# Queries with no matching key: scale and bias zero in the exponential, in place of a mean of v made by GpSimd and TensorE

## What is computed

```
q_bits = (q @ proj > 0);  k_bits = (k @ proj > 0)
mask = q_bucket[:, :, :, None] == k_bucket[:, :, None, :]
scores = where(mask, q @ k.T / sqrt(D), -1e9)
scores = scores - max(scores, axis=-1)
attn = exp(scores)
attn = attn / (sum(attn, axis=-1) + 1e-9)
out = attn @ v
```

## Time and profile before

| | |
|---|---|
| median of 3 runs | 767.33 us (766.6 to 768.45) |
| profiled execution, time | 768.82 us |
| its span, first to last instruction | 767.0 us |
| busy: TensorE, VectorE, ScalarE, GpSimd | 656.2, 425.9, 341.4, 340.7 us |
| attention in the span | 0 to 276 us |
| mean granted TensorE clock | 0.924 of full |

### The profile page before, as it was taken

The page is one execution under the profiler, slowest core; times in us unless marked ns, Lnnn a source line. Parts: engine busy times, 40 slices in busy tenths (PEclk is TensorE's granted clock), DMA queues, the critical chain, the costliest instruction groups (busy, mean ns, idle before and its releaser), DMA issues. The chain is left out here.

```text
span 767.0 us, 10365 instructions
## 1 busy us (share of the span) xinstructions
PE 656.2 (86%) x3758; PEld 521.2 (68%) x3759; DVE 425.9 (56%) x568; ACT 341.4 (45%) x528; POOL 340.7 (44%) x204
## 2 busy tenths in 40 slices
PE   2999999999999879108799999999576899889998
PEld 0666666666666569108699998898455688668886
DVE  6877787877875321604265545661169884632222
ACT  2766666766656623005055533451245463612200
POOL 4573753936632046253266444660156545723300
PEclk9999999999999975557899999999878999989999
DMA  9105162360632045145565667711352202122311
GB/s 302 42 1 171 42 214 73 142 208 6 212 132 109 1 184 199 71 178 170 189 228 201 210 213 244 246 44 41 109 194 71 68 0 83 41 83 83 109 42 56
DMA packets 50975, 96.09 MB, mean 125 GB/s; under 512 B 16624, under 2 KB 16624, under 8 KB 50928
## 3 DMA queue, kind: packets, MB, share of 16 engines
q1 hardware_dynamic: 48720, 88.38, 33.7%
q0 software_dynamic: 1920, 6.29, 2.3%
q10 hardware_dynamic: 288, 0.79, 0.3%
HBM read 69.23 MB, written 26.21 MB: 124 GB/s over the span
## 5 line engine op out<-in xcount | busy, mean ns | idle before, releaser
L879 POOL TENSOR_TENSOR w_lo<-stage,w_hi 128x1024 fp32r<-128x1024 f32 x28 | 85.1, 3058 | 92.0 <-ACT w_hi L874 92.0
L250 ACT COPY probs_t<-turned 128x768 f32<-128x768 f32 x96 | 76.8, 800 | 68.4 <-PE turned L427 63.5
L312 DVE TENSOR_REDUCE neg_max<-scores 128x1 f32<-128x768 f32 x96 | 91.6, 955 | 26.4 <-PE scores L418 24.5
L258 ACT ACTIVATE probs<-scores,neg_max 128x768 f32<-128x768 f32 x96 | 86.9, 905 | 23.4 <-DVE neg_max L312 23.3
L427 PE MATMUL turned<-ident,probs 128*128 128x128 f32 x576 | 80.7, 276 | 13.7 <-ACT probs_t L250 13.6
L427 PEld LDWEIGHTS turned<-ident,probs 128*128 128x128 f32 x576 | 65.6, 142 | 29.8 <-issue 28.2
L968 PE MATMUL up<-xt_hi,w_hi 128*128 128x256 f32 x256 | 75.7, 296 | 7.7 <-issue 5.7
L968 PE MATMUL up<-xt_hi,w_lo 128*128 128x256 f32 x256 | 75.0, 293 | 0.0
L968 PE MATMUL up<-xt_lo,w_hi 128*128 128x256 f32 x256 | 75.0, 293 | 0.0
L439 PE MATMUL pv<-probs_t,v_in 128*64 128x384 f32 x384 | 72.3, 498 | 0.8 <-DVE out_t L319 0.8
L418 PE MATMUL scores<-k_aug,q_aug 76*128 76x384 f32 x192 | 59.7, 393 | 9.5 <-DVE k_aug L305 8.7
(11 more groups left out here) (170 smaller groups left out, 1420.8 us busy)
## 6 DMA issues: line engine op xcount, KB each, us to landing
stage<-in_w SPq DMA_DIRECT2D x64, 512.0 KB, 4.6
wt_raw<-in_w_tok SPq DMA_DIRECT2D x12, 768.0 KB, 4.5
x_slots<-zeros SPq DMA_DIRECT2D x7, 1024.0 KB, 8.6
y_slots<-zeros SPq DMA_DIRECT2D x7, 1024.0 KB, 10.4
q_raw<-in_qT SPq DMA_DIRECT2D x16, 384.0 KB, 5.2
k_raw<-in_kT SPq DMA_DIRECT2D x14, 384.0 KB, 5.8
x_in<-x_slots SPq DMA_DIRECT2D x10, 512.0 KB, 5.1
y_slots<-y_out SPq DMA_DIRECT2D x8, 512.0 KB, 2.8
```

The source lines that it names most:

```text
L250: nc.scalar.copy(probs_t[j % 2][:, a, :, t % 3 * P:(t % 3 + 1) * P].rearrange("k (b n) q -> k b n q", b=2), turned[:, :, 0:HALF].rearrange ...
L258: nc.scalar.activation(probs[g % 3][:].rearrange("p (b n) -> p b n", b=2), scores[g % 2][:, :, 0:HALF], ACT.Exp, bias=neg_max[:, pair, a, ...
L312: nc.vector.tensor_reduce(neg_max[:, pair, a, t:t + 1], scores[g % 2][:, :, 0:HALF], AX.XY, ALU.max, negate=True).then_inc(s_max, 1)
L879: name.tensor_tensor(w_lo[w][:, r, :], stage[:, r, :], w_hi[w][:, r, :].bitcast(F32), ALU.subtract).then_inc(done, 1)
```

## The change

`exponential` gets a scale for each query beside the bias. After each `maximum` VectorE makes two values for each query: `match` (1 where the maximum is above `FLOOR`, else 0) and `bias` (`neg_max` times the same). For a query without a match the exponential is then exp(0 * score + 0) = 1 for every key, its sum 768, and the ordinary path gives the mean of v. `maximum` signals a new semaphore, `s_neg`, for which VectorE itself waits before the two small instructions; `s_max` counts those two. Everything that made and added the mean goes: `sum_v`, `add_fallback`, the matmul with `ones`, `v_mean`, `no_match`, the multiplication in `reciprocals`, and their buffers, semaphores and waits.

```diff
@@ -58,18 +58,14 @@
     q_hl = of_heads("q_hl", [P, S], F32R)
     k_lh = of_heads("k_lh", [P, S], F32R)
     v_in = [sb(f"v_in{p}", [P, 2, T, D]) for p in range(2)]
-    v_add = sb("v_add", [P, 2, 3, D])
-    v_sum = sb("v_sum", [P, 2, D])
-    v_mean = sb("v_mean", [P, 2, D])
-    fallback = sb("fallback", [P, T, 2, D])
     probs = [sb(f"probs{n}", [P, S]) for n in range(3)]
     probs_t = [sb(f"probs_t{n}", [P, 2, T, HALF]) for n in range(2)]
     out_t = [sb(f"out_t{n}", [P, HALF]) for n in range(2)]
     neg_max = sb("neg_max", [P, NPAIRS, 2, T])
     total = sb("total", [P, NPAIRS, 2, T])
-    no_match = sb("no_match", [P, 2, T])
+    match = sb("match", [P, NPAIRS, 2, T])
+    bias = sb("bias", [P, NPAIRS, 2, T])
     recip = sb("recip", [P, 2, T])
-    ones = sb("ones", [P, P])
     proj_raw = sb("proj_raw", [P, NBITS])
     w_bits = sb("w_bits", [P, 2 * NBITS])
     thresh = [sb("thresh_q", [P, 1]), sb("thresh_k", [P, 1])]
@@ -140,7 +133,7 @@
         for pair in range(2):
             load_v(pair)
         load_routing(sp)
-        sp.wait_ge(s_constp, 4)
+        sp.wait_ge(s_constp, 3)
         for n in range(2):
             clear(sp, None, n)
         for pair in range(NPAIRS):
@@ -158,7 +151,6 @@
                     clear(sp, pair - 1, n)
             if pair + 2 < NPAIRS:
                 sp.wait_ge(s_pv, 2 * pair + 2)
-                sp.wait_ge(s_vadd, 3 * pair + 1)
                 load_v(pair + 2)
 
     @block.gpsimd
@@ -167,7 +159,6 @@
         pool.wait_ge(s_constp, 1)
         nc.gpsimd.affine_select(out=ident[:], in_=ident[:], compare_op=ALU.not_equal, fill=1.0, base=0,
                                 pattern=[[-1, P]], channel_multiplier=1).then_inc(s_constp, 1)
-        nc.gpsimd.memset(ones[:], 1.0).then_inc(s_constp, 1)
         nc.gpsimd.memset(zeros[:], 0.0).then_inc(s_constp, 1)
 
         def q_high(pair, a):
@@ -191,30 +182,6 @@
                 pool.wait_ge(s_khi, 2 * pair + a + 1)
             nc.gpsimd.tensor_tensor(k_lh[p][a][0:D, :], k_raw[p][a][0:D, :], k_aug[p][a][0:D, :].bitcast(F32),
                                     ALU.subtract).then_inc(s_klo, 1)
-
-        def sum_v(pair):
-            p = pair % 2
-            pool.wait_ge(s_klo, min(2 * pair + 4, NHEADS))
-            pool.wait_ge(s_v[p], 32 * (pair // 2) + 32)
-            nc.gpsimd.tensor_tensor(v_add[:], v_in[p][:, :, 0:3, :], v_in[p][:, :, 3:6, :], ALU.add).then_inc(s_vadd, 1)
-            pool.wait_ge(s_vadd, 3 * pair + 1)
-            nc.gpsimd.tensor_tensor(v_add[:, :, 0, :], v_add[:, :, 0, :], v_add[:, :, 1, :], ALU.add).then_inc(s_vadd, 1)
-            pool.wait_ge(s_vadd, 3 * pair + 2)
-            if pair > 0:
-                pool.wait_ge(s_vmean, pair)
-            nc.gpsimd.tensor_tensor(v_sum[:], v_add[:, :, 0, :], v_add[:, :, 2, :], ALU.add).then_inc(s_vadd, 1)
-
-        def add_fallback(pair):
-            pool.wait_ge(s_vmean, pair + 1)
-            pool.wait_ge(s_rec, 4 * pair + 4)
-            if pair > 0:
-                pool.wait_ge(s_x, pair)
-            nc.gpsimd.tensor_tensor(fallback[:], v_mean[:].unsqueeze(1).to_broadcast([P, T, 2, D]),
-                                    no_match[:].rearrange("q a t -> q t a").unsqueeze(3).to_broadcast([P, T, 2, D]),
-                                    ALU.mult).then_inc(s_fall, 1)
-            pool.wait_ge(s_fall, pair + 1)
-            pool.wait_ge(s_norm, 2 * pair + 2)
-            nc.gpsimd.tensor_tensor(x_of(pair), x_of(pair), fallback[:], ALU.add).then_inc(s_x, 1)
 
         k_low(0, 1)
         pool.wait_ge(s_qhi, 2)
@@ -227,10 +194,6 @@
                     q_high(pair + 1, a)
                     k_high(pair + 1, a)
                     k_low(pair + 1, a)
-            sum_v(pair)
-            if pair > 0:
-                add_fallback(pair - 1)
-        add_fallback(NPAIRS - 1)
 
     @block.scalar
     def _(act):
@@ -252,11 +215,11 @@
 
         def exponential(g):
             pair, a, t = place(g)
-            act.wait_ge(s_max, g + 1)
+            act.wait_ge(s_max, 2 * g + 2)
             if g >= 3:
                 act.wait_ge(s_tp, g - 2)
             nc.scalar.activation(probs[g % 3][:].rearrange("p (b n) -> p b n", b=2), scores[g % 2][:, :, 0:HALF], ACT.Exp,
-                                 bias=neg_max[:, pair, a, t:t + 1],
+                                 bias=bias[:, pair, a, t:t + 1], scale=match[:, pair, a, t:t + 1],
                                  accum_out=total[:, pair, a, t:t + 1]).then_inc(s_exp, 1)
 
         for g in range(STEPS + TURN_LAG):
@@ -310,7 +273,13 @@
             pair, a, t = place(g)
             dve.wait_ge(s_sc, g + 1)
             nc.vector.tensor_reduce(neg_max[:, pair, a, t:t + 1], scores[g % 2][:, :, 0:HALF], AX.XY, ALU.max,
-                                    negate=True).then_inc(s_max, 1)
+                                    negate=True).then_inc(s_neg, 1)
+
+            dve.wait_ge(s_neg, g + 1)
+            nc.vector.tensor_scalar(match[:, pair, a, t:t + 1], neg_max[:, pair, a, t:t + 1], -FLOOR, None,
+                                    ALU.is_le).then_inc(s_max, 1)
+            nc.vector.scalar_tensor_tensor(bias[:, pair, a, t:t + 1], neg_max[:, pair, a, t:t + 1], -FLOOR,
+                                           neg_max[:, pair, a, t:t + 1], ALU.is_le, ALU.mult).then_inc(s_max, 1)
 
         def evict_out(j):
             dve.wait_ge(s_pv, j + 1)
@@ -322,23 +291,14 @@
             dve.wait_ge(s_exp, 12 * pair + 12)
             if pair > 0:
                 dve.wait_ge(s_norm, 2 * pair)
-                dve.wait_ge(s_fall, pair)
             nc.vector.tensor_scalar_add(recip[:], total[:, pair, :, :], 1e-9).then_inc(s_rec, 1)
-            nc.vector.tensor_scalar(no_match[:], neg_max[:, pair, :, :], -FLOOR, 1.0 / S, ALU.is_gt, ALU.mult).then_inc(s_rec, 1)
-            dve.wait_ge(s_rec, 4 * pair + 1)
+            dve.wait_ge(s_rec, 2 * pair + 1)
             nc.vector.reciprocal(recip[:], recip[:]).then_inc(s_rec, 1)
-            dve.wait_ge(s_rec, 4 * pair + 3)
-            nc.vector.scalar_tensor_tensor(recip[:], neg_max[:, pair, :, :], -FLOOR, recip[:], ALU.is_le,
-                                           ALU.mult).then_inc(s_rec, 1)
 
         def normalise(j):
             pair, half = divmod(j, 2)
             dve.wait_ge(s_ot, j + 1)
-            dve.wait_ge(s_rec, 4 * pair + 4)
-            if half == 0:
-                if pair > 0:
-                    dve.wait_ge(s_fall, pair)
-                nc.vector.tensor_copy(v_mean[:].rearrange("q a d -> q (a d)"), side[:, HALF:512]).then_inc(s_vmean, 1)
+            dve.wait_ge(s_rec, 2 * pair + 2)
             tiles = slice(3 * half, 3 * half + 3)
             nc.vector.tensor_tensor(x_of(pair, tiles), side[:, 0:HALF].rearrange("q (t a d) -> q t a d", t=3, a=2),
                                     recip[:, :, tiles].rearrange("q a t -> q t a").unsqueeze(3).to_broadcast([P, 3, 2, D]),
@@ -399,7 +359,6 @@
             j = max(0, (g - TURN_LAG + 5) // 6)
             if j > 0:
                 pe.wait_ge(s_norm, j)
-                pe.wait_ge(s_vmean, (j + 1) // 2)
 
         def score(g):
             pair, a, t = place(g)
@@ -443,15 +402,12 @@
 
         def turn_out(j):
             pe.wait_ge(s_oev, j + 1)
-            if j % 2 == 0:
-                pe.wait_ge(s_vadd, 3 * (j // 2) + 3)
-                nc.tensor.matmul(side[:, HALF:512], ones[:], v_sum[:].rearrange("p a d -> p (a d)"), start=True, stop=True)
             for n in range(3):
                 last = nc.tensor.transpose(side[:, n * P:(n + 1) * P], out_t[j % 2][:, n * P:(n + 1) * P], ident[:])
             last.then_inc(s_ot, 1)
 
         pe.wait_ge(s_const, N_CONSTS)
-        pe.wait_ge(s_constp, 3)
+        pe.wait_ge(s_constp, 2)
         for a in range(2):
             pe.wait_ge(s_qk[0][a], 32)
             for of_k in range(2):
```

More of the change, by code:

```diff
@@ L96, in attention @@
     s_sc = sem("s_sc")
+    s_neg = sem("s_neg")
     s_max = sem("s_max")
@@ L105, in attention @@
     s_norm = sem("s_norm")
[L106 to L109, removed]
     block = ctx.enter_context(nc.Block())
```

## The result

The changed kernel takes 756.25 us (median of 4 runs, 755.32 to 756.76); the kernel before took 767.84 us beside it. The ratio is 0.9848, 95% interval 0.9832 to 0.9864: 11.6 us faster, where 2.1 us were forecast and the range ended at 762.8. The profiled execution took 756.28 us.

A forecast was written before the change was run, and what follows sets the result against it. TensorE was taken to pace attention, with later stages untouched. The terms -2.2 - 1.95 + 0.9 + 1.1 were summed to -2.1 us, giving 765.3 us on the median of 767.33; the range was 762.8 to 771.5.

The forecast's parts named there:

- Mean's matmuls: TensorE in attention: turning out without the mean's matmul saves 0.27 us for each of 8 pairs, 2.2 us.
- Last addition: End of attention: GpSimd's last addition of the mean, all on the path, goes and saves 1.95 us.
- Start: Start of attention: TensorE waits for each exponential, so delays from the small instructions aren't hidden; 1.1 us lost, between 0.4 and 2.1.
- Ends of pairs: Step 11 of a pair: small instructions held behind GpSimd's L177 delay the waiting score, 0.15 us at six places, 0.9 us.
- first rival: VectorE's one-element instructions are not held while GpSimd works; all but 0.4 us is covered, 763.6 us; chance 0.18.
- The reading that both kinds are held: VectorE in attention: both kinds of small instruction, seen held with 12 elements, wait until GpSimd's instruction is over.
- second rival: GpSimd's next instruction starts before VectorE's second small one, which waits up to 2.3 us more; 769.7 to 774 us; chance 0.25.
- the third: Rival: the two small instructions cost VectorE 0.5 us, not 0.27, in each step; +3.3 us, 768.6 us; chance 0.15.
- Second operand of the exponential: ScalarE in attention: a scale from memory beside the bias adds between 0 and 0.11 us to each exponential, taken as 0.1.

The follow-up runs named there:

- cheaper bias: The changed kernel with the bias made by tensor_scalar with two scalars in place of scalar_tensor_tensor, same values; 756.37 us (ratio 0.9856).
- changed + 47: The changed kernel with 94 satisfied waits (47 instructions) behind routing's last matmul, in TensorE's idle time; 764.48 us (ratio 0.9959).
- first try: The changed kernel with 47 satisfied waits (24 instructions by the page) at the head of the experts' TensorE program; 760.92 us (ratio 0.9903).
- with the matmul: The changed kernel with one unread TensorE matmul of the mean's shape before every second turning-out, 16 instructions more; 763.89 us (ratio 0.9936).

## Why the prediction was wrong

The step that failed is this one: "The stages after attention start when its last engine is done and are not touched: what attention gains or loses is what the program does." Attention gained 3.5 us and the experts 8.4, and the latter through the number of instructions that stand ahead of them in TensorE's program. That is shown both ways: 47 idle instructions make the changed kernel's stage 8.8 us longer, 209 make that of the kernel before 9.5 us shorter. The forecast costed every instruction that goes by its duration and none by its place. What would have made the forecast wrong was named ("so does a later stage that changes its own length"), without a rival or a chance for it, although the row with 3.97 us of idle time for "issue" stood in the trace of before.

The sum itself is -2.15 us and so 765.2 us, written as -2.1 and 765.3. Its terms, by the table above:

- **Mean's matmuls, -2.2: right.** First to last eviction fell by 2.26 us; the matmul alone brings 2.20 back. Where the earlier trace rows had 0.57 us to the next score there are now 0.31.
- **Last addition, -1.95: right,** 1.98. The kernel before without that addition alone has 2.40 us from the last eviction to the end, 1.72 less; the other 0.25 goes with the rest of GpSimd's last wait. The next stage follows 0.33 us after the last normalisation (0.34 forecast):

```profile
273.02 0.56 DVE L303 TENSOR_TENSOR x_all<-side,recip 128x384 f32<-128x384 f32 x1 [0.70 <-PE side L406]
...
273.91 1.07 PE L704 MATMUL banks<-ident,x_all 128*128 128x128 f32 x8 [0.93 <-PEq L1365]
```

- **Start, +1.1: 0.6 to 0.9.** The first exponential starts at 20.87 in place of 20.27, the second at 22.00 in place of 21.55. The first eviction comes 0.8 us later than in the kernel before and 0.9 later than without the small instructions, but it moves by up to 0.9 us between traces of one kernel, roughly with the moment at which the granted clock rises to 1.00; where that moment is 26.6 to 26.8 us, the difference is 0.6 to 0.7 (50.25 before, 50.80 and 50.94 changed).
- **Ends of pairs, +0.9: nothing.** A pair takes 31.05 us, 0.29 less than in the earlier trace rows and just the mean's share (31.07 was given for the case that all is covered); without the small instructions first to last is the same 220.5.

```profile
113.33:144.38 31.05, 29.76 (x191) 19.48 (x192) 26.55 (x55) 21.79 (x37) 11.73 (x9) 1.00 0.41 132
```

The term took the small instructions of step 11 to be held behind L177, L168 in the changed kernel. There they are not held, and the exponential starts 0.29 us after its maximum, in place of the 1.35 reckoned with (138.0 to 139.35). Timeline of GpSimd, VectorE and ScalarE:

```profile
137.37 2.43 POOL L168 TENSOR_SCALAR q_hl<-q_raw 128x768 fp32r<-128x768 f32 x1 [18.53 <-PE scores L377]
137.84 0.96 DVE L275 TENSOR_REDUCE neg_max<-scores 128x1 f32<-128x768 f32 x1
138.83 0.15 DVE L279 TENSOR_SCALAR match<-neg_max 128x1 f32<-128x1 f32 x1
138.91 0.15 DVE L281 SCALAR_TENSOR_TENSOR bias<-neg_max 128x1 f32<-128x1 f32 x1
139.09 0.99 ACT L221 ACTIVATE probs<-scores,bias,match 128x768 f32<-128x768 f32 x1 [0.19 <-DVE bias L281]
```

So it is in all 7 places where `bias` starts within L168 (148 to 150 ns each). Being held is real, but elsewhere: `match` is never held (153 to 155 ns, 96 times), `bias` 19 times in 96, three in each of six pairs and one at the start, 15.9 us in all, 13 times behind L183 and 6 behind the cast L174. The longest kind:

```profile
117.03 1.82 POOL L183 TENSOR_TENSOR k_lh<-k_raw,k_aug 64x768 fp32r<-64x768 f32 x1 [0.15 <-POOL k_lh L176]
117.19 0.15 DVE L279 TENSOR_SCALAR match<-neg_max 128x1 f32<-128x1 f32 x1
117.26 1.60 DVE L281 SCALAR_TENSOR_TENSOR bias<-neg_max 128x1 f32<-128x1 f32 x1
118.90 0.95 DVE L260 SCALAR_TENSOR_TENSOR q_hl<-q_raw,q_hl 64x768 fp32r<-64x768 f32 x1
118.90 0.99 ACT L221 ACTIVATE probs<-scores,bias,match 128x768 f32<-128x768 f32 x1 [1.09 <-DVE bias L281]
```

`bias` ends as GpSimd's L183 ends, 118.86 against 118.85, and the exponential is over a microsecond late; ScalarE's slack takes it. With the bias by tensor_scalar none is held (at most 0.21 us), and attention is no shorter. So the first rival (not held) was half right in its premise and right in its effect on the pairs; its figure for attention, -3.75 us, was the nearest to what was measured. The reading that both kinds are held was right for 12 elements, also in the other pairs before (344 to 347 ns in five of them behind L177, in place of 164 to 174), and did not carry over to one. The second rival, GpSimd getting in between, did not happen: the longest hold is 1.60 us and ends with the instruction it waits for. Nor did the third: where nothing holds them, VectorE has both values 0.26 us after the maximum (138.80 to 139.06), not 0.5. The Trainium skill, page "SBUF — State Buffer", section "SBUF: two separate sides", names VectorE operations with two SBUF inputs, against a GpSimd one that reads SBUF, among those that take an exclusive lock. The rows behind L183 and L174 agree with it; those within L168, which reads SBUF too, do not.

- **Second operand of the exponential, 0.1: right,** 994 ns in place of 905, +0.09. The Trainium skill's 93 ns (page "ScalarE: Activation LUTs", section "What ACT_TABLE_LOAD costs") agrees.

The sum of attention's terms is -3.5 against -2.1 forecast, the difference being the pairs' ends and a part of the start. Had attention been all, the forecast would have been off by 1.4 us; what put the time outside its range is the experts' stage.

What stays open: routing's -0.96. It goes with the moment at which the granted clock falls to 0.50 after attention, which differs between kernels: at 275.6 to 276.0 us (cheaper bias, changed + 47, first try) routing takes 68.6 to 68.9 us, at 278.1 (before) 68.36, at 280.7 (changed) 67.40, at 282.7 (with the matmul) 65.82. What sets that moment I did not test, and I don't count it as a gain of the change. Open as well is what fills a stall of 4 us when the block's load takes 1 us, and with it whether TensorE waits for its code at all. The stall before runs from 374.36 to 378.33, with one load over at 374.49 and the next begun at 378.14; in the first try it runs from 371.82 to 376.57, and the next load begins at 377.52, after it. The runs show that the stalls follow the number of instructions ahead, with a period of 256, and not how. The trace has weight and token transfers on the same engines at those times, and I ran nothing that takes them away.

## What to carry to other kernels

Before costing a change to one stage, look in the others for idle time of the pacing engine that ends in nothing visible: near a branch it can depend on how many instructions stand ahead, and any edit of that engine's program re-draws it, here by up to 10.8 us, more than the edit itself. To tell the two apart, put as many harmless instructions back in a place where the engine idles, and count them in the page's instruction total. A kernel with such a loop is worth a few runs with different padding: the changed kernel with the cheaper bias and 128 instructions of padding, 755.81 us, is the fastest that computes everything, though within the noise of the change itself (756.25), while the kernel before had 8 us to gain from 209.

## What the runs showed of the hardware

- TensorE's stalls at the loop over the experts were none, 0.6 to 1.9, or 3.8 to 4.8 us long, by the number of its instructions ahead, and came back with a period of 256 instructions (stage 204.91 us with 256 added, 204.84 with none; 213.26 and 213.62 at the same offset in two kernels).
- A stall of 3.8 us or more came with 3.4 to 6.8 us at 1.2 GHz in the dense matmuls behind it, those of 1.76 to 1.85 us by 3.4 us, those of 1.64 us and less by none; in the kernel before the clock roughly doubled what the stalls cost (3.9 us beside 4.1).
- Two satisfied waits in a row made one instruction of TensorE, and one such came every 0.11 us (256 hidden ones reached from 315.03 to 342.73 us). They are free only as long as the idle time lasts.
- A one-element tensor_scalar on VectorE was never held by GpSimd, with one scalar from memory or an immediate; scalar_tensor_tensor was, for up to 1.60 us, behind GpSimd's two-tensor L183 (13 of 13) and its cast L174 (6 of 6), and not within its tensor_scalar L168 (0 of 7). With 12 elements a tensor_scalar was held within GpSimd's tensor_scalar L177 of the kernel before (344 ns in place of 164 to 174).
